# The second layer's experts computed inside the capacity search

## The reference

```python
order = np.argsort(-flat)
for idx in order:
    tok, e = (int(idx) // E, int(idx) % E)
    if assigned[tok] >= 0 or counts[e] >= cap:
        continue
    assigned[tok] = e
    counts[e] += 1
...
for e in range(E):
    mask = assigned == e
    h = np.maximum(x[mask] @ w1[e], 0.0)
    out[mask] = h @ w2[e]
```

## Time and profile before

| | |
|---|---|
| median of 3 runs | 1203.68 us (1199.72 to 1204.15) |
| the profiled execution's own time | 1199.88 us |
| its span, first to last instruction | 1198.1 us |
| PE busy | 925.9 us (77%) |
| DVE busy | 569.3 us (48%) |
| ACT busy | 324.3 us (27%) |
| POOL busy | 228.3 us (19%) |
| mean granted clock of PE | 0.862 of 2.4 GHz |

### The profile page before, as it was taken

The page is one execution under the profiler, slowest core; times in us unless marked ns, Lnnn a source line. Parts: engine busy times, 40 slices in busy tenths (PEclk is TensorE's granted clock), DMA queues, the critical chain, the costliest instruction groups (busy, mean ns, idle before and its releaser), DMA issues.

```text
span 1198.1 us, 23541 instructions
## 1 busy us (share of the span) xinstructions
PE 925.9 (77%) x7460; PEld 761.5 (64%) x7461; DVE 569.3 (48%) x1602; ACT 324.3 (27%) x659; POOL 228.3 (19%) x339
## 2 busy tenths in 40 slices
PE   5999999258999999999943332222269999999995
PEld 4787787246888888888832222222158888888883
DVE  5766657663222222222236677777734444445431
ACT  2555445052222222222230000000023443434420
POOL 5643332011111211112110000000012222222220
PEclk9999999569999999999975555555579999999998
DMA  9668673444111111111111000000023543445300
GB/s 186 132 129 169 122 150 67 154 167 168 36 35 35 44 44 35 35 35 35 44 27 67 0 0 0 0 0 0 0 97 115 185 164 125 147 152 184 114 30 24
DMA packets 45988, 97.48 MB, mean 81 GB/s; under 512 B 7248, under 2 KB 19584, under 8 KB 45952
## 3 DMA queue, kind: packets, MB, share of 16 engines
q1 hardware_dynamic: 27200, 59.55, 17.2%
q0 software_dynamic: 8064, 26.46, 6.7%
q10 hardware_dynamic: 10688, 11.01, 4.6%
HBM read 77.49 MB, written 19.51 MB: 81 GB/s over the span
## 4 chain that ended last, share of the span: by engine, by line
PE 62%; issue 26%; DVE 6%; POOL 2%; DMA 2%; ACT 1%; DVEq 0%; ACTq 0%; SPq 0%; POOLq 0%
PE bank L688 43%; PE bank L600 3%; PE bank L712 3%; PE bank L581 3%; PE bank L641 2%; PE bank L695 2%; PE bank L735 2%; PE bank L618 2%; PE bank L590 1%; DMA q_eye<-in_q 1%; PE bank L728 1%; PE bank L632 1%; DVE ksum L1016 1%; ACT W L896 1%; DVE W L1210 1%
## 5 line engine op out<-in xcount | busy, mean ns | idle before, releaser
L688 PE MATMUL bank<-W,xh 128*128 (+1 forms) x784 | 253.8, 405 | 13.4 <-DVE gates L1216 10.6
L688 PE MATMUL bank<-W,hh 128*128 (+1 forms) x784 | 253.0, 404 | 11.6 <-DVE hl L1223 11.6
L688 PEld LDWEIGHTS bank<-W,xh 128*128 128x128 f32 x784 | 145.7, 191 | 45.9 <-issue 11.2
L688 PEld LDWEIGHTS bank<-W,hh 128*128 128x128 f32 x784 | 145.8, 191 | 44.0 <-issue 10.3
L688 PE MATMUL bank<-W,hl 128*128 (+1 forms) x392 | 156.4, 399 | 0.0
L688 PE MATMUL bank<-W,xl 128*128 (+1 forms) x392 | 155.9, 398 | 0.0
L779 PE MATMUL bank<-ge,cb 128*8 128x16 bf16 x1344 | 42.3, 172 | 106.6 <-DVE ge L1335 106.6
L1223 DVE TENSOR_TENSOR hl<-bank,hh 128x512 fp32r<-128x512 f32 x98 | 63.1, 686 | 96.9 <-ACT hh L896 91.5
L779 PEld LDWEIGHTS bank<-ge,cb 128*8 128x8 bf16 x1344 | 36.1, 83 | 111.9 <-DVE ge L1335 111.9
L896 ACT ACTIVATE xh<-bank 128x512 fp32r<-128x512 f32 x50 | 29.8, 595 | 268.5 <-PE bank L695 268.5
L520 POOL COPY sidx<-idx 128x1 int32 (+1 forms) x49 | 27.3, 556 | 368.4 <-DVE y L1231 249.2
(11 more groups left out here) (238 smaller groups left out, 1322.8 us busy)
## 6 DMA issues: line engine op xcount, KB each, us to landing
raw_w<-in_moe_w SPq DMA_DIRECT2D x20, 2048.0 KB, 9.4
va<-in_v_win SPq DMA_DIRECT2D x16, 585.0 KB, 6.3
k_raw<-in_k SPq DMA_DIRECT2D x16, 384.0 KB, 9.4
q_eye<-in_q ACTq DMA_DIRECT2D x16, 384.0 KB, 7.2
x_rows<-x ACTq DMA_DIRECT2D x12, 384.0 KB, 9.1
x_rows<-x SPq DMA_DIRECT2D x4, 387.0 KB, 7.2
xg<-x_rows,gidx POOLq DMA_INDIRECT x26, 3.4
y_rows<-y,sidx POOLq DMA_INDIRECT x25
```

What stands on the lines that cost most here:

```text
L688: last = mm(ps, lhs[a][:, c, :], rhs[b](c), start=c == 0 and t == 0, stop=c == n - 1 and t == 2)
```

## The change

The second layer is made one pipeline of ten passes, written out without loops. Pass `ph` runs the search phase `ph` (the first seven passes), prepares the expert shut in the pass before (`r = ph - 1`: its list of rows, the gather of its 384 rows, the split of its weights), and computes the products of the one before that (`q = ph - 2`). Experts are taken in the order in which they are shut. PE's and DVE's programs lay pieces of the three jobs between each other by hand: a pass has 28 segments (`SEG`), 16 of the first product (6 matmuls each) and 12 of the second, and three of them stand in each of the 8 search steps.

Other parts: the first product is now turned round, with the weights held still and 384 rows moving, so that the hidden values come out turned and 8 transposes a tile go away; the list of an expert's rows is made on POOL (`picks`, 50 small chained instructions) and by one group of 24 matmuls (`list_mine`); the low parts of the second layer's weights are made by POOL and no longer by DVE (`low_parts`); `build_slots(1)` goes away; ACT copies the results out of PSUM. In the first layer only the early load of expert 0's weights moves ahead of the last store of `x`.

```diff
+STEPS = 32 // 4
+PH = E - 1
+SEG = 3 * STEPS + 4
+UPS = 2 * FC
+RANKS_AT, LIST_AT = 1, 5
...
+            def load_second(r):
+                sp.wait_ge(eid_ready, r + 1)
+                e = sp.value_load(eids[0:1, r:r + 1], min_val=0, max_val=E - 1)
+                if r >= 2:
+                    sp.wait_ge(hidden_done, FC * (r - 1))
+                sp.dma_start(w1_at[:, r % 2, :, :], w1b[bass.ds(e, 1), :, :].rearrange("o (c p) f -> p (o c) f", p=P)).then_inc(w1_in[r % 2], 16)
...
+            def picks(r):
+                pool.wait_ge(places_ready, r + 1)
+                if r:
+                    pool.wait_ge(listed, r)
+                wide = lambda a, n: a.unsqueeze(2).to_broadcast([P, TC, n])
+                for j in range(TC):
+                    chain2(g.tensor_scalar(slot_hot[:, j, :], iota_l[:, :], mlo[:, j:j + 1], mine[:, j:j + 1], ALU.is_equal, ALU.mult))
+                    chain2(g.tensor_scalar(mtile[:, j, :], iota_t[:, 0:GT], mhi[:, j:j + 1], None, ALU.is_equal))
+                chain2(g.tensor_tensor(msel[:, :, 0, :], mtile[:, :, :], iota_p[:, :].unsqueeze(2).to_broadcast([P, TC, GT]), ALU.mult))
+                chain2(g.tensor_tensor(msel[:, :, 1, :], mtile[:, :, :], wide(iota_j[:, :], GT), ALU.mult))
+                g.nop().then_inc(picks_ready, 1)
+
+            def low_parts(r, units):
+                for u in units:
+                    pool.wait_ge(high_done, (W1U + W2U) * r + u + 1)
...
+                    g.tensor_tensor(low, whole, high.bitcast(F32), ALU.subtract).then_inc(low_done, 1)
...
+            for ph in range(E + 2):
+                q, r = ph - 2, ph - 1
+                if 0 <= r < E:
+                    picks(r)
+                    for t in range(GT):
+                        gather_second(r, t)
+                    low_parts(r, range(W1U))
+                if q >= 0:
+                    store_second(q, 0)
+                if 0 <= r < E:
+                    low_parts(r, range(W1U, W1U + W2U))
+                if q >= 0:
+                    store_second(q, 1)
+                    store_second(q, 2)
...
+            def hidden(q, fc, half):
+                if fc == 0 and half == 0:
+                    pe.wait_ge(xlow_done, GT * (q + 1))
+                    pe.wait_ge(low_done, (W1U + W2U) * q + W1U)
+                if half == 0 and FC * q + fc >= 2:
+                    pe.wait_ge(hlow_done, FC * q + fc - 1)
+                f = slice(P * fc, P * fc + P)
+                for c in range(KC // 2 * half, KC // 2 * half + KC // 2):
+                    for t, (w, a) in enumerate(((w1h, xh2), (w1h, xl2), (w1l, xh2))):
+                        last = mm(bank[fc % 2][:, 0:CAP], w[:, q % 2, c, f], a[:, c, :], start=c == 0 and t == 0, stop=c == KC - 1 and t == 2)
+                if half:
+                    last.then_inc(hidden_done, 1)
...
+                for t in range(STEPS):
+                    if ph < PH:
+                        count(ph, t)
+                    segment(3 * t)
+                    if t == RANKS_AT and 0 <= r < E:
+                        rank_mine(r)
+                    if ph < PH:
+                        any_full(ph, t)
+                    segment(3 * t + 1)
+                    if t == LIST_AT and 0 <= r < E:
+                        list_mine(r)
+                    segment(3 * t + 2)
+                if ph < PH:
+                    count_found(ph)
+                segment(SEG - 4)
+                if ph < PH:
+                    spread_rows(ph)
+                segment(SEG - 3)
+                if ph < PH:
+                    rank_ties(ph)
+                segment(SEG - 2)
+                if ph < PH:
+                    count_taken(ph)
+                segment(SEG - 1)
...
+            for ph in range(E + 2):
+                q, r = ph - 2, ph - 1
...
+                if ph < PH:
+                    prepare(ph)
+                for t in range(STEPS):
+                    if ph < PH:
+                        compare(ph, t)
+                    lows_until(3 * t)
+                    if t == 0 and 0 <= r < E:
+                        mark_mine(r)
+                    if ph < PH:
+                        mark_full(ph, t)
+                    if t == RANKS_AT and 0 <= r < E:
+                        place_mine(r)
+                    if ph < PH:
+                        next_digit(ph, t)
+                    if t == LIST_AT and 0 <= r < E:
+                        take_list(r)
+                    if t == STEPS - 1 and 0 <= r < E:
+                        rows_low(r, 0)
+                if ph < PH:
+                    find(ph)
+                if 0 <= r < E:
+                    rows_low(r, 1)
+                if ph < PH:
+                    choose(ph)
+                    shut(ph)
+                if 0 <= r < E:
+                    rows_low(r, 2)
```

More of the change, by code:

```diff
@@ L254, in two_layers_of_experts @@
[L254 to L265, removed]
@@ L564, in _ @@
+            for t in range(GT):
+                pool.wait_ge(out_stored[t], 16 * E)
         @block.tensor
@@ new lines, in outward @@
+            def outward(q, t, part):
+                if part == 0:
+                    if t == 0:
+                        pe.wait_ge(low_done, (W1U + W2U) * (q + 1))
+                    if GT * q + t >= 2:
+                        pe.wait_ge(out_copied, GT * q + t - 1)
+                if t == 0:
+                    pe.wait_ge(hlow_done, FC * q + 2 * part + 2)
+                rows = slice(P * t, P * t + P)
+                for c in range(2 * part, 2 * part + 2):
+                    for n, (a, w) in enumerate(((hh2, w2h), (hh2, w2l), (hl2, w2h))):
+                        last = mm(bank[2 + t % 2][:, :], a[:, c, rows], w[:, q % 2, c, :], start=c == 0 and n == 0, stop=c == FC - 1 and n == 2)
+                if part == 3:
+                    last.then_inc(out_done, 1)
@@ new lines, in turn_rows, with segment @@
+            def turn_rows(r, t):
+                pe.wait_ge(rows_in[t], 16 * (r + 1))
+                pe.wait_ge(xlow_done, GT * r + t)
+                for c in range(KC):
+                    last = tr(bank[4][:, P * c:P * c + P], xg2[t][:, P * c:P * c + P], ident[:, :])
+                last.then_inc(rows_turned, 1)
+            for ph in range(E + 2):
+                q, r = ph - 2, ph - 1
+                def segment(k):
+                    if k < UPS:
+                        if q >= 0:
+                            hidden(q, k // 2, k % 2)
+                    else:
+                        t, part = (k - UPS) // 4, (k - UPS) % 4
+                        if q >= 0:
+                            outward(q, t, part)
+                        if part == 3 and 0 <= r < E:
+                            turn_rows(r, t)
+                for t in range(STEPS):
[22 more added lines that the diff above has]
+                segment(SEG - 1)
@@ L1289, in _ @@
             chain.start(base)
-            for u in range(W1U):
-                split_lo(1, u, 0, 0)
+            chain = Chain(dve, dve_chain2)
             chain(vec.memset(free[:, :], 1.0))
@@ new lines, in _, with compare @@
+            kb = known[:, 0:1].to_broadcast([P, KSEARCH])
+            def compare(ph, t):
+                if t in (1, 2):
+                    finite(thr[:, :])
+                tf = (thr if t else thr0)[:, :].bitcast(F32).unsqueeze(1)
+                for half in range(2):
+                    r = slice(TC // 2 * half, TC // 2 * half + TC // 2)
+                    tt(ge[:, r, :], smx[:, r].unsqueeze(2).to_broadcast([P, TC // 2, KSEARCH]),
+                       tf.to_broadcast([P, TC // 2, KSEARCH]), ALU.is_ge).then_inc(ge_ready, 1)
+                if t >= 2:
+                    chain(stt(known[:, :], digit[:, :], 4 * (t - 1) - 3, known[:, :], ALU.logical_shift_right, ALU.bitwise_xor))
+                if 1 <= t < STEPS - 1:
+                    chain(tt(nxt[:, :], digits[:, t + 1, :], kb, ALU.bitwise_xor))
```

452 lines of the change are left out of this document (264 added, 188 removed).

## The result

The changed kernel takes 1332.1 us (median of 4 runs, 1327.3 to 1333.7) where the kernel before, measured beside it, takes 1202.25: 1.1075 times as long, with a 95% interval of 1.1037 to 1.1112. The forecast was 1186 us and faster, so its sign was wrong. The profiled execution took 1331.6 us, its span 1329.7.

The account below looks back on a forecast made before the run. Search was bound by latency, products by PE. First count at 631.5, passes 31.3 + 62 + 5 x 66 - 2.8 + 43 + 43 + 46.3 give 1184.3, with 1.8 outside 1186 us, against 1199.9; range 1108 to 1232.

Parts of the forecast that it names:

- PE late at the list: PE waits at `list_mine`: 2.7 us in a full pass, 10 in pass 1, 3 each in passes 7 and 8.
- low parts' hold on DVE: POOL's subtractions, 2.0 us each in two runs of four, delay DVE's search: 9.3 us a full pass, 14 in pass 1.
- the rest: The forecast sum without late list and low parts' hold; a full pass is then 54 us.
- A pair with two scalar operands: In POOL's picks, one pair of chained instructions takes 0.60 us, bounds 0.54 and 0.85; 50 instructions take 15 us.
- ready at 29: The expert's list is ready 29 us into a pass; PE arrives at 26.5, so it waits 2.7 us.
- the rival of the late list: Slower picks delay PE: 19 us in eight passes per 0.1 us a pair; 1234 us at 0.85; chance 0.20.
- the surcharge of 5 us: About 25 DVE operations fall between POOL's picks, 0.2 us each, lengthening the picks from 15 to 20 us.
- PE's line: PE's work in a pass with all three jobs is 45 us, 384-column matmuls taking 0.18 us each.
- the 2000 rows in one line: A condition that would refute the forecast: PE's program, some 2000 rows written out, not arriving in time.
- The border: Between passes, last transposes, copies, `prepare` and the first `ge` take 5.3 us, 0.4 covered: PE waits 4.9 us.
- POOL's hold on DVE: A POOL instruction holds out DVE operations with two SBUF inputs until it ends; beside picks, 0.1 to 0.2 us each.
- The clock: Rival: PE's clock falls at each border, costing 3 us a pass in five and 4 later, 1205 us; chance 0.13.

Follow-up runs that it names:

- experiments 1 to 3: Changed kernel with, in turn: picks on DVE, 1212.5 us; no low parts made (output lacks their correction), 1256.9 us; both edits, 1137.2 us.
- experiment 3: Changed kernel with picks on DVE and no low parts made (output lacks their correction): 1137.2 us, 0.9423 of the kernel before.
- Experiment 12: Changed kernel with unread filler matmuls in PE's waits: 24 at the border of passes 3 to 6, 64 ahead of the list in passes 2 to 8: 1315.6 us.
- experiment 9: Kernel with picks and low parts on DVE, plus 24 unread matmuls in PE's wait at the border of passes 3 to 6: 1132.0 us.
- experiments 3 and 8: 8: changed kernel with picks and low parts on DVE, ACT's order changed so high parts are ready: 1142.1 us, 0.9492 of the kernel before. 3: see experiment 3.
- experiments 8 and 11: 11: experiment 8's kernel, third row tile's low part behind the next pass's first comparison, 10 unread matmuls at borders of passes 3 to 6: 1125.9 us, 0.9338.
- experiment 4: Changed kernel with POOL's low parts each made in four pieces of 256 columns, waiting for each piece's end: 1298.5 us.
- experiment 10: Kernel with picks and low parts on DVE, the third row tile's low part moved behind the next pass's first comparison: 1130.1 us.

## Why the prediction was wrong

The sum on record taken apart, beside what was measured (low parts and list by experiments 1 to 3, which agree both ways; these two rows hold the lower clock behind their waits too):

| | on record | measured |
|---|---|---|
| PE late at the list, all passes | 2.7 x 5 + 10 + 3 + 3 = 29.5 | 120 |
| low parts' hold on DVE | 9.3 x 5 + 14 = 60.5 | 75 |
| the rest (1186 - 90; experiment 3) | 1096 | 1137 |
| in all | 1186 | 1332 |

**The step that failed** is the size of one term: "A pair with two scalar operands I take as 0.60 us (bounds 0.54, and 0.85 if a second operation doubles the cost by column)". A pair takes 1.30, above the upper bound. The chained POOL instructions of the earlier trace rows that it was scaled from have no scalar by partition; with one, a comparison of 128 columns takes 0.63 us, a second operation adds 0.19, and even three columns take 0.31. So the list, "ready at 29", is ready 868.83 - 824.62 = 44 us into the pass, and PE is there at 31 (12.88 earlier) instead of 26.5. (The terms on record for PE's arrival, 5 x 4.2 + 0.7 + 1.08 + 1.40, come to 24.2 and not 26.5; the wait for `place_mine` of 1.5 may be part of the rest. In the trace the fourth and fifth steps take 4.3 us as forecast, and the first three, with the lower clock in them, 7.1, 5.7 and 6.2.) The mechanism was on record as the rival of the late list, with the right slope, 19 us for each 0.1 us: 0.70 us over the 0.60 is 134 us by it, on top of the 29.5. Off go 33 us, since the surcharge of 5 us for DVE's operations between the pairs came at 0.9 in the pass shown (three comparisons of 24 took longer). That makes 131; PE's waits at the list are 129.3, and the run without the chain shows 120. The rival's chance of 0.20 was too low and its end, 1234, came from a bound of 0.85 that no row supported.

This term is the largest error but not the only one. With it right and the rest of the sum as on record, the forecast would have been 1186 + 90 = 1276 us, slower than before. With the list as on record and the other two rows as measured, it would have been 1332 - 90 = 1242 us, slower too: the 15 us more of the low parts and the 41 of the rest undo the forecast gain by themselves.

**PE's line** held where the clock did: hidden matmuls 0.17 us apart (0.18 on record), outward 0.23, and the first count waits for DVE's `ge` behind `prepare`. In the view of PE's waits from 660 us on every row names another engine or a DMA and none the program itself, so the 2000 rows in one line arrived in time.

**The border** of 4.9 us is 4.53. `ge` alone took 0.35 us a half, as said. Pass 0 took 32.0 us for 31.3.

**POOL's hold on DVE** held for the low parts and its price nearly so: 2.37 us for 2.0 a part. The Trainium skill's GPSIMD Engine Reference, section 3.1, led to an estimate of 2.2, and stood nearer. It did not hold for the picks: the forecast let each DVE operation wait 0.1 to 0.2 us beside them, and `ge` there keeps its 0.63 us for two halves, with a `slot_hot` begun 0.31 us before it. "An instruction of the one holds the other out until it ends" is thus shown for POOL's subtraction and for the copy of the earlier trace rows, not for its comparison. That "DVE gets one SBUF operation in for each POOL instruction" is true only with a gap between POOL's instructions, or for the pair of parts at 893.69; in the runs of four and six DVE waited for the last. Why it got in between the two at 893.69, which show no gap either, stays open. One difference is in the rows: the four high parts of the long run were ready long before it (854.68 + 3.88), while the second of these two was ready only at 894.56, when POOL had begun the first; that this is the cause, no run shows. Section 8 of the same page (the Trainium skill), which names the contention but no length, agrees with the low parts' rows; beside the picks the only sign of it is the three longer comparisons. In time the two forms of the hold differ less than their look: one operation of 8.27 us in a run, against waits of up to 2.4 with gaps, and 15 us in the whole kernel.

**The clock** had a rival of its own, at each border, 0.13. It was no rival but a companion: behind the waits at the border, at the list and beside the low parts it was low each time, 0.78 to 0.80 granted for about 0.9 on record. It was low behind a short wait of 1.24 us for the third count too: from 838.5 to 841.7 hidden matmuls are 0.32 us apart. Experiment 12 gives 16.5 us for eleven of these waits; the rival had said 19. The page TensorE: Matmul & The Clock Gate (the Trainium skill), section HAM oscillation, warned of bursts with waits between, and the trace agrees.

**The rest**, 41 us above the record, lies in the passes: in the kernel of experiment 3 a full one takes 60.5 us (mean of the four from 710.8 to 953.0) where the record has 54 without the two losses, and the first with a list 44.6 for 38.3. PE is busy for 51.5 to 51.8 us of such a pass, granted 0.91, where its line on record is 45, all at the upper level. Some 10 us are clock at four borders (experiment 9). DVE's own picks, some 5 us of work a pass that this kernel has and the record has not, may be much of what is left; how much of them is on the path was not measured.

Where the gain went, then: with both jobs off POOL a pass takes 60 us (experiments 3 and 8), where a phase took 32.6 and an expert's products 306.7 / 8 = 38, and the kernel is 5 to 7% faster than before (experiments 8 and 11). The merging itself pays; what the change put on POOL beside it cost more than the merging brings.

## What to carry to other kernels

Price an instruction only from a row of its own form on its own engine, scalar operands included; where none exists, let the upper bound be far, and multiply it by the length of the chain before choosing the likeliest case. A small engine that is idle is not free: see who waits in order behind its last instruction, and whom its instructions hold out while they run. Where the time moves 19 us for 0.1 us of one small instruction, and the gain is gone at 0.09 above its estimate, the late case deserves about as large a chance as the one in time.

## What the runs showed of the hardware

- POOL's TENSOR_SCALAR with scalars by partition: 0.31 us for 3 columns, 0.63 for 128 with one operation, 0.80 with two. DVE's comparison of 768 columns, six such rows, takes 0.95.
- POOL's subtraction of two SBUF operands: 0.73 us for 256 columns (experiment 4), 2.37 for 1024.
- DVE's `ge`, which reads two SBUF operands, is not held by POOL's comparison (0.63 us for its two halves with and without it); a comparison that begins just behind a `ge` takes 1.04 to 1.20 us instead of 0.80.
- DVE was held through four and six POOL instructions that followed one another without a gap, 8.27 and 11.39 us in one operation, the second in the first pass with a list:

```profile
708.62 13.84 POOL L628 TENSOR_TENSOR w_low<-w_landed,w_high 128x1024 fp32r<-128x1024 f32 x6
```

```profile
711.08 11.39 DVE L1539 SCALAR_TENSOR_TENSOR known<-digit,known 128x1 int32<-128x1 int32 x1
```

- PE's clock fell about 2 us after the end of a wait of only 1.95 us, in a stretch that also had light matmuls (experiment 10); with fillers in a wait of 4.5 us it stayed up, granted 1.00 for 0.60 in the 43 matmuls behind (experiment 9).
